# Weights of the second network: split during attention, or split in the routing head and the first expert

## The reference, cut to what matters

```python
for t in range(S):                              # _attn_ref: B, H, S, D = 4, 8, 768, 48
    cur = np.einsum('bhd,bhe->bhde', u[None] * kt, vt)
    y[:, :, t] = np.einsum('bhd,bhde->bhe', rt, state + cur)
    state = w[None, :, :, None] * state + np.einsum('bhd,bhe->bhde', kt, vt)
x = y.transpose(0, 2, 1, 3).reshape(3072, 384)
# _moe_ref: 8 experts take 384 tokens each, in the order of falling logits
for e in range(8):
    out[mask] = np.maximum(x[mask] @ w1[e], 0.0) @ w2[e]      # 384x1024, 1024x384
# _moe2_ref, on every token
h = np.maximum(x @ w_in, 0.0)                   # 384x2048
return h * h @ w_out                            # 2048x384
```

## Time and profile before

| | |
|---|---|
| median of 3 executions | 878.4 us (878.37 to 878.81) |
| the profiled execution | 878.33 us |
| its span, from first to last instruction | 876.6 us |
| mean granted clock of TensorE | 0.969 |
| attention, until the first routing instruction | 168.65 us |
| first matmul of the first expert | at 212.99 us |

### The profile page before, as it was taken

How to read it: one execution, slowest core, us unless ns; L and a number is a source line. 1 busy time by engine, 2 the same in 40 slices (tenths; PEclk the granted TensorE clock), 3 DMA queues, 4 the chain that set the end, 5 groups by cost and what they waited for, 6 DMA issues and landing times.

```text
span 876.6 us, 18438 instructions
## 1 busy us (share of the span) xinstructions
PE 811.8 (93%) x6695; PEld 777.4 (89%) x6695; DVE 551.1 (63%) x1159; ACT 290.0 (33%) x581; POOL 328.7 (37%) x312
## 2 busy tenths in 40 slices
PE   5999999624999999999999999999999999999995
PEld 4888888623899999999999999999999999999995
DVE  7999999675777458546845692678358633931210
ACT  1233332103135315422542253235314533542332
POOL 6777677203026303520541063126303520531232
PEclk9999999855999999999999999999999999999998
DMA  8776776013023001200310040022002200400000
GB/s 228 213 220 232 214 250 209 29 51 121 2 73 100 26 2 72 99 27 0 120 50 27 8 162 0 27 72 99 9 18 72 99 27 1 172 1 28 1 1 27
DMA packets 22143, 69.86 MB, mean 80 GB/s; under 512 B 3552, under 2 KB 6752, under 8 KB 22112
## 3 DMA queue, kind: packets, MB, share of 16 engines
q1 hardware_dynamic: 19040, 59.99, 21.2%
q0 software_dynamic: 3072, 9.44, 3.1%
HBM read 59.98 MB, written 9.44 MB: 79 GB/s over the span
## 4 chain that ended last, share of the span: by engine, by line
PE 77%; DVE 11%; issue 5%; POOL 5%; ACT 1%; DMA 0%; DVEq 0%; POOLq 0%
PE bank L1196 16%; PE bank L1197 15%; PE bank L1198 15%; PE bank L1250 8%; PE bank L1252 8%; PE bank L1251 8%; PE bank L1143 3%; DVE ks L638 2%; PE bank L1059 2%; DVE am L645 1%; DVE rs L639 1%; POOL rku L401 1%; DVE hot L802 1%; POOL kn L385 1%; POOL rk L396 1%
## 5 line engine op out<-in xcount | busy, mean ns | idle before, releaser
L469 POOL TENSOR_TENSOR h_lo<-sq,h_hi 128x384 fp32r<-128x384 f32 x128 | 152.9, 1198 | 398.2 <-DVE sq L966 398.1
L966 DVE SCALAR_TENSOR_TENSOR sq<-bank,relu 128x384 f32<-128x384 f32 x128 | 71.0, 555 | 133.6 <-ACT relu L565 133.3
L1250 PE MATMUL bank<-m_hi,h_hi 128*128 128x384 f32 x384 | 132.0, 344 | 0.0
L1196 PE MATMUL bank<-x_hi,m_hi 128*128 128x384 f32 x384 | 130.6, 340 | 0.3
L1252 PE MATMUL bank<-m_hi,h_lo 128*128 128x384 f32 x384 | 129.8, 338 | 0.0
L1251 PE MATMUL bank<-m_lo,h_hi 128*128 128x384 f32 x384 | 129.5, 337 | 0.0
L1197 PE MATMUL bank<-x_lo,m_hi 128*128 128x384 f32 x384 | 129.2, 336 | 0.0
L1198 PE MATMUL bank<-x_hi,m_lo 128*128 128x384 f32 x384 | 129.1, 336 | 0.0
L565 ACT ACTIVATE relu<-bank 128x384 f32<-128x384 f32 x128 | 63.0, 492 | 194.5 <-PE bank L1198 192.3
L559 ACT ACTIVATE h_hi<-bank 128x384 fp32r<-128x384 f32 x64 | 31.5, 492 | 192.1 <-PE bank L1198 192.0
L958 DVE SCALAR_TENSOR_TENSOR h_lo<-bank,h_hi 128x384 fp32r<-128x384 f32 x64 | 35.4, 554 | 72.0 <-ACT h_hi L559 72.0
(11 more groups left out here) (172 smaller groups left out, 1572.4 us busy)
## 6 DMA issues: line engine op xcount, KB each, us to landing
w_raw<-we_in SPq DMA_DIRECT2D x48, 512.0 KB, 4.9
nn<-nn_in SPq DMA_DIRECT2D x24, 576.0 KB, 4.1
tt<-tt_in SPq DMA_DIRECT2D x48, 192.0 KB, 4.9
m_raw<-m_in SPq DMA_DIRECT2D x12, 512.0 KB, 5.7
x_rows<-yrow SPq DMA_DIRECT2D x24, 192.0 KB, 1.9
xg<-x_rows,perm_next POOLq DMA_INDIRECT x24, 4.4
out<-xg,perm_now POOLq DMA_INDIRECT x24, 2.6
u_row<-u_in SPq DMA_DIRECT2D x1, 192.0 KB, 6.0
```

Of the source, the lines that this page charges most:

```text
L469: pool.tensor_tensor(h_lo[g % 3][:, :], sq[g % 2][:, :], h_hi[g % 3][:, :].bitcast(f32), ALU.subtract).then_inc(lo2_ready, 1)
L966: dve.scalar_tensor_tensor(out=sq[g % 2][:, :], in0=h_ps[g % 3][:, 0:CAP], scalar=0.0, in1=relu[:, :], op0=ALU.max, op1=ALU.mult).then_inc ...
L1196: pe.matmul(out, hi_w, hi_x, start=first, stop=False)
L1250: pe.matmul(acc_ps[t][:, 0:DM], h_hi[r][:, s], m2_hi[:, c:c + DM], start=first, stop=False)
```

## The change

The second network's tiles are no longer split in attention. All twelve are loaded once into a tile `m2_raw` that occupies the same memory as `m2_lo`, so that the low part is written over the loaded values. The six tiles of `w_in` are loaded after the last rows of attention are stored, the six of `w_out` after the loads of the first expert. The high parts are made by ScalarE: three before it splits the first expert's weights, three after its `x_high`, six at hidden tiles 2, 3, 4, 9, 10 and 11 of the first expert. The low parts of `w_in` are made by GpSimd: four as soon as `x_lo` is complete, two at hidden tiles 8 and 10. Those of `w_out` are made by VectorE at hidden tiles 8, 10, 13, 16, 18 and 21. TensorE waits for them where it first uses them. The first expert is written out ahead of the loops of GpSimd, ScalarE and VectorE.

```diff
+IN_TILES = [d * (F2 // WT) + f for f in range(F2 // WT) for d in range(DC)]
+OUT_TILES = list(range(DC * F2 // WT, M2_TILES))
+IN_LOW_AT = {8: 4, 10: 5}
+OUT_HIGH_AT = {2: 0, 3: 1, 4: 2, 9: 3, 10: 4, 11: 5}
+OUT_LOW_AT = {8: 0, 10: 1, 13: 2, 16: 3, 18: 4, 21: 5}
...
+        m2_raw = sb("m2_raw", [P, M2_TILES * WT], f32, loaded)
+        loaded.close()
+
         m2_lo = sb("m2_lo", [P, M2_TILES * WT], f32r)
...
+        def m2_high(eng, j):
+            cols = slice(j * WT, (j + 1) * WT)
+            eng.wait_ge(m2_loaded[j], 16)
+            return eng.activation(m2_hi[:, cols], m2_raw[:, cols], ACT.Copy)
+        def m2_low(eng, j):
+            cols = slice(j * WT, (j + 1) * WT)
+            return eng.tensor_tensor(m2_lo[:, cols], m2_raw[:, cols], m2_hi[:, cols].bitcast(f32), ALU.subtract)
...
-                elif b < 3:
-                    load_m2(b - 1, b - 1)
...
-                    if not last and b % 2:
-                        sp.wait_ge(m2_lo_ready, 4 * i + b + 1)
-                        load_m2(b // 2, 2 * i + b // 2 + 2)
...
+            for j in IN_TILES:
+                load_m2(j)
             sp.wait_ge(logit_ready, NU)
             load_expert(0)
+            for j in OUT_TILES:
+                load_m2(j)
...
+            def in_low(n):
+                pool.wait_ge(in_hi_ready, n + 1)
+                m2_low(pool, IN_TILES[n]).then_inc(in_lo_ready, 1)
+            pool.wait_ge(x_lo_ready, DC)
+            for n in range(len(IN_TILES) - len(IN_LOW_AT)):
+                in_low(n)
...
                     if not last and g == GATHER_AT:
                         gather(i + 1)
+                    if is_first(i) and g in IN_LOW_AT:
+                        in_low(IN_LOW_AT[g])
...
-                    if b % 2 and not (last and b == B - 1):
-                        m2_high(2 * i + b // 2 + 1, 1 - b // 2, i + 1 + b // 2)
...
+            for j in IN_TILES[0:DC]:
+                m2_high(act, j).then_inc(in_hi_ready, 1)
             for j in range(W1_TILES + 1):
                 split_high(0, j)
             for d in range(DC):
                 x_high(0, d)
+            for j in IN_TILES[DC:]:
+                m2_high(act, j).then_inc(in_hi_ready, 1)
...
                     high(i, g)
+                    if is_first(i) and g in OUT_HIGH_AT:
+                        m2_high(act, OUT_TILES[OUT_HIGH_AT[g]]).then_inc(out_hi_ready, 1)
...
-                    m2_low(i, b)
...
+            def out_low(n):
+                dve.wait_ge(out_hi_ready, n + 1)
+                m2_low(dve, OUT_TILES[n]).then_inc(out_lo_ready, 1)
...
+                        if is_first(i) and g in OUT_LOW_AT:
+                            out_low(OUT_LOW_AT[g])
...
                 pe.wait_ge(masked, 2 * n + 2)
+                pe.wait_ge(nn_in[b], 16 * i + 16)
...
+                        if (g - G1) * P % WT == 0 and d == 0:
+                            pe.wait_ge(in_lo_ready, DC * ((g - G1) * P // WT + 1))
...
                     pe.wait_ge(lo2_ready, G2 * i + g - G1 + 1)
+                    tiles = [-(-k * DM // WT) for k in (g - G1, g - G1 + 1)]
+                    if tiles[0] < tiles[1]:
+                        pe.wait_ge(out_lo_ready, tiles[1])
...
-            pe.wait_ge(m2_lo_ready, 2 * M2_TILES)
```

More of the change, by code:

```diff
@@ L106, in build @@
         m2_hi = sb("m2_hi", [P, M2_TILES * WT], f32r)
+        loaded = ExitStack()
+        m2_raw = sb("m2_raw", [P, M2_TILES * WT], f32, loaded)
+        loaded.close()
         m2_lo = sb("m2_lo", [P, M2_TILES * WT], f32r)
@@ L153, in build @@
         wg = sb("wg", [P, DC, E], f32, att)
-        m2_raw = [sb(f"m2_raw{j}", [P, WT], f32, att) for j in range(2)]
         att.close()
@@ L225, in build @@
         inter_done = sem("inter_done")
-        m2_in = [sem(f"m2_in{j}") for j in range(2)]
         scores_ready, masked, update_ready, z_ready = sem("scores_ready"), sem("masked"), sem("update_ready"), sem("z_ready")
@@ L231, in build @@
         yT_sum, yT_ready, logit_sum, logit_ready = sem("yT_sum"), sem("yT_ready"), sem("logit_sum"), sem("logit_ready")
-        m2_hi_ready, m2_lo_ready = sem("m2_hi_ready"), sem("m2_lo_ready")
+        m2_loaded = [sem(f"m2_loaded{j}") for j in range(M2_TILES)]
+        in_hi_ready, in_lo_ready = sem("in_hi_ready"), sem("in_lo_ready")
+        out_hi_ready, out_lo_ready = sem("out_hi_ready"), sem("out_lo_ready")
         y_stored = [sem(f"y_stored{b}") for b in range(B)]
@@ L278, in load_nn, with load_m2 @@
                 sp.dma_start(nn[b][:, :, :], nn_d[bass.ds(n, 1), :, :, :].rearrange("o p a f -> p (o a) f")).then_inc(nn_in[b], 16)
-            def load_m2(j, n):
-                sp.dma_start(m2_raw[j][:, :], m2_d[bass.ds(n, 1), :, :].rearrange("o p f -> p (o f)")).then_inc(m2_in[j], 16)
+            def load_m2(j):
+                sp.dma_start(m2_raw[:, j * WT:(j + 1) * WT], m2_d[j, :, :]).then_inc(m2_loaded[j], 16)
             sp.wait_ge(w_gap, 1)
@@ L481, in expert @@
                     keep_perm(i + 1)
-            with pool.Fori(0, E - 1) as i:
+            expert(0, False)
+            with pool.Fori(1, E - 1) as i:
                 expert(i, False)
@@ L492, in _ @@
             act.sem_inc(out_ready, TT)
-            def m2_high(m, j, times):
-                act.wait_ge(m2_in[j], 16 * times)
-                act.activation(m2_hi[:, bass.ds(m * WT, WT)], m2_raw[j][:, :], ACT.Copy).then_inc(m2_hi_ready, 1)
             def turned_y(n):
@@ L526, in units @@
                         gated(n - 1)
-                    if b % 2 and not (last and b == B - 1):
-                        m2_high(2 * i + b // 2 + 1, 1 - b // 2, i + 1 + b // 2)
-            m2_high(0, 0, 1)
             units(0, False)
@@ L589, in _ @@
                 split_high(0, j)
-            with act.Fori(0, E - 1) as i:
+            expert(0, False)
+            with act.Fori(1, E - 1) as i:
                 expert(i, False)
@@ L665, in state_sum @@
                                   u_ps[0:HD, 0:PAIRS * D].rearrange("p (q f) -> p q f", q=PAIRS), ALU.add).then_inc(z_ready, 1)
[L667 to L673, removed]
             def rows(i, b):
@@ L1024, in _ @@
                 split_low(dve, 0, j)
-            with dve.Fori(0, E - 2) as i:
+            expert(0, False, True)
+            with dve.Fori(1, E - 2) as i:
                 expert(i, False, True)
```

## The result

The changed kernel takes 880.5 us (median of 8 executions, 880.27 to 881.53), the kernel before 878.4 (8 executions, 878.29 to 878.81): ratio 1.0027, 95% interval 1.0016 to 1.0037. It is 2.1 us slower; 882.4 was predicted, in a range of 877.5 to 886.0. The executions fall into two groups, five at 880.3 to 880.5 and three at 881.5. The profiled one is of the upper group (881.5 us, span 879.8, mean clock 0.961), so its trace accounts for 3.2 us more than the span before, not for 2.1. The mean clock of the lower five is 0.964, of the upper three 0.961, 0.961 and 0.963.

What follows compares the result with a forecast made beforehand. Attention was taken as bound by a VectorE-GpSimd chain containing `m_lo`, with TensorE the busy engine from the routing head on. Terms: 5.2 + 2.3 + 4.8 + 0.6 - 8.9 = +4.0 us on 878.4, so 882.4 us, range 877.5 to 886.

Steps and rivals of the forecast that it cites:

- likeliest case: The forecast itself, chance 0.58: attention gains, the first expert loses more, 882.4 us; alone it reaches from 880.3 to 885.
- attention: Attention units: without `m_lo` TensorE becomes the bound, gaining 8.9 us (8.1 to 9.4).
- routing head: Routing head: input loads and three `m_hi` fall in ScalarE's idle time; cost 0.
- wait for `h_lo` at the start: First expert's start: GpSimd's four subtractions hold VectorE, so TensorE idles 6.2 us instead of 1.0; +5.2 us (4.7 to 5.9).
- first fall of the clock: First expert's start: TensorE's long idle drops its clock to 0.50, with a slow return; +2.3 us (0 to 3.4).
- second half, VectorE's chain: First expert's second half: two GpSimd and two VectorE pieces delay the next expert's list; +4.8 us (2.5 to 6).
- `h_lo` of tile 15: First expert's second half: GpSimd's `h_lo` behind the late gather comes late; +0.6 us (0 to 1.5).
- the rival with the full clock: First expert's start: the chip does not count the 6.2 us as idle, clock stays full; 880.1 us, chance 0.17.
- the bound over VectorE and GpSimd: Attention unit: the chain over both engines without `m_lo` would take 6.35 - 0.56 = 5.79 us.
- the rule that VectorE is held for the sum of GpSimd's pieces: First expert's start: VectorE's two-input work waits out GpSimd's four pieces, 2.28 us each, 9.1 us, until 223.0.
- GpSimd lets VectorE through: First expert: GpSimd's subtractions are held up instead of holding VectorE, start costs 0, no clock fall; 870 us, chance 0.12.
- attention does not shorten: Attention: units stay at 6.35 us because `rku` goes before `ks`; 891 us, chance 0.08.

Runs made afterwards that it cites:

- e5: Changed kernel with 42 extra matmuls (results unused) keeping TensorE busy ahead of its second `contract` of the first expert; 880.0 us.
- e1: Changed kernel with GpSimd's four input-tile subtractions at the first expert's start moved to VectorE's wait for the gathered rows; 876.3 us.
- e6: Changed kernel with only VectorE's first two output pieces moved, from hidden tiles 8 and 10 to 4 and 5; 878.7 us.
- e4: Kernel before with VectorE's attention subtraction `m_lo` replaced by a one-input reduction over as many values, low parts left out; 869.2 us.
- e7: Changed kernel with only GpSimd's last two input pieces (hidden tiles 8 and 10) moved to VectorE's wait for the gathered rows; 876.8 us.
- e10: Changed kernel rearranged: VectorE's `w_lo` wait for the first gather's landing; GpSimd splits two input tiles afterwards, VectorE four by tile 7, outputs from tile 4; 867.6 us.
- e3: Changed kernel with four input pieces on VectorE before the gathered rows, two on GpSimd after keeping the row list, first two output pieces at tiles 4, 5; 870.4 us.
- e9: Kernel before with one line more: VectorE's three `w_lo` ahead of the first expert wait until the first gather has landed; 876.9 us.
- e11: e10 with the first `w_lo` moved from GpSimd, where it ran beside `hot`, to VectorE behind `hot`; 866.2 us.

## Why the prediction was right, and where its sizes were off

The likeliest case happened, at its lower edge. By its steps, for the profiled execution:

| step | predicted | measured | from |
|---|---|---|---|
| attention | -8.9 | -9.0 | shift at the first tile |
| routing head | 0 | 0 | same |
| wait for `h_lo` at the start | +5.2 | +4.7 | e5: -9.0 to -4.3 |
| first fall of the clock | +2.3 | +1.3 | e5 against the changed kernel, fourth tile |
| second half, VectorE's chain | +4.8 | +4.6 | starts of TensorE, -3.0 to +1.6; the same in e1 and e5 |
| `h_lo` of tile 15 | +0.6 | 0 | no wait there; 0.5 in e1, e5 and e6, where the clock stays full |
| second fall of the clock | none | +1.6 | starts of TensorE, +1.6 to +3.2 |
| sum | +4.0 | +3.2 | spans 879.8 and 876.6 |

That the trace comes as near as 0.8 us to the forecast is luck in part: the second fall, which the forecast did not have, makes up for terms that were too large. Without it the measured steps are -9.0, +4.7, +1.3 and +5.1, in all +2.1, which is also the difference of the medians. The stated range held; the sum was 1.9 us too high. The median of 880.5 lies only 0.4 us from the 880.1 of the rival with the full clock; it is the trace that decides against that rival, not the time.

**Attention** went as worked out: `ownv` 0.83 us, 5.86 us per unit, TensorE the bound. e4 shows the reason: an instruction of the same length with one input costs nothing. Of the bound over VectorE and GpSimd (5.79 us) nothing can be said, since TensorE's lies above it.

**The start**: the rule that VectorE is held for the sum of GpSimd's pieces held. 5.2 was too much by 0.5 because I counted all of VectorE's time behind 208.7 us as blocked; `best` with one input runs beside the last piece (0.34 us), so that much was not lost. The rest I leave unexplained.

**The clock**: the likeliest case was right that it falls, and 2.3 us for it was the mis-sized term. It is at 0.50 from 217 to 223.8 us, but TensorE stands idle until 218.5 of that. Both traces begin the second `contract` there, and until the end of the group for tile 3 the changed kernel's matmuls are slower by 2.0 us: the nine of the `contract` take 3.05 us in place of 1.71, the group of tile 3 takes 2.68 in place of 2.00. But in e5 TensorE waits for VectorE's `hot` between the two (0.36 us in the line shown; with the matmuls that follow it 0.7 us), and the changed kernel comes too late to wait. 2.0 less 0.7 is the 1.3. The second fall was not in the forecast at all: three waits of 1.71, 0.76 and 1.24 us within 14 us, ahead of a fall at 268.2. It comes and goes: e1 and e5 have the same waits for VectorE, and their profiled executions do not have it; what decides it stays open. The Trainium skill's page TensorE: Matmul & The Clock Gate (section HAM oscillation), by which a wait between blocks of matmuls can make the next block start cold, agrees with the changed kernel's trace at the first place, where one wait of 5.17 us stands ahead of the slow matmuls. The three shorter waits of the second place are not the case which that section describes.

**The second half**: 4.6 us against 4.8, and its division was right in place: 1.9 us at the ranks, 2.4 at the ids, and 0.4 ahead of both, which the sum did not have: VectorE's piece at tile 8 holds GpSimd's `h_lo`. The sum took 4.56 us of GpSimd's pieces and 2.28 of VectorE's together, less 1.4 of idle time and 0.65 of slack. By the same sum GpSimd's alone would cost 2.5 us (3.1 with the `h_lo` of tile 15) and VectorE's alone 0.2; measured are 3.4 and 0.7 (e6, e7), so each alone was set too low and the two together too high. The 0.6 for the `h_lo` of tile 15 is there as 0.5 in e1, e5 and e6; in the changed kernel's trace TensorE comes there late by its fallen clock and does not wait.

**The rivals.** That GpSimd lets VectorE through is refuted by `gt` at 2.33 us and `pre` at 2.40. That attention does not shorten is refuted by its 5.86 us; the order of `ks` and `rku` did not flip. That the clock stays full did not happen, but e5, in whose trace it does, has its fastest executions at 879.0 to 879.3, where that rival had been given 880.1.

## What to carry to other kernels

Where VectorE and GpSimd both work on SBUF, count the two as one resource. On VectorE's side this held here for instructions with two SBUF inputs and for `gt`, whose second input is a column of scalars, but not for reductions; on GpSimd's side for its subtractions, for a small copy and for the issue of a gather. Look for a short instruction that lasts as long as its neighbour on the other engine. Where VectorE has such work waiting, a piece on the idle GpSimd costs VectorE twice what the same piece costs on VectorE itself (2.3 us against 1.14 for 128x1024), so moving it pays only where VectorE has nothing of this kind to do, and the same goes for VectorE beside the issue of a gather. An edit that wins time in a balanced stage must put its work where the engine it holds is waiting: the same twelve subtractions cost 12 us in the first expert as placed by the change (2.9 of it by the clock), and nothing in e10, where the shift stays at -10.8.

## What the runs showed of the hardware that I had not expected

**VectorE holds the issue of GpSimd's indirect transfers.** Beside VectorE's two-input `w_lo` the issues take 2.05 and 1.77 us, beside `m_lo` 1.97 (e3); with VectorE idle they take 1.15, 0.95 and 0.95 (e9). One line that makes VectorE wait is worth 1.5 us in the kernel before.

**A small instruction is held as long as a large one.** `gt`, a TENSOR_SCALAR of 128x24 with a column of scalars, took 2.33 us beside GpSimd's `m_lo`, and a GpSimd copy of 128x3 took 1.02 to 1.11 us beside VectorE's `w_lo` (e9, e10, e11; 0.18 us otherwise). Reductions, with one input, were not held: `best` took 0.34 us beside `m_lo`, and `scrap` of e4 0.68 beside `ownv`.

**The two engines take turns.** At the start of the changed kernel the four GpSimd pieces took 2.38, 2.38, 3.38 and 3.32 us and VectorE's two `w_lo` 1.93 and 3.42: each of the last two pieces waited for one `w_lo` of 1.1 us, and the second `w_lo` waited for one piece of 2.3.

**The same waits do not always bring a fall of the clock.** The changed kernel's trace has one from 268.2 to 271.6 us, which costs 1.1 us net; the traces of e1 and e5 have the same waits for VectorE and no fall. That equal executions of one kernel differ in this way is likely by the two groups of the changed kernel, 1.2 us apart with mean clocks of 0.964 and 0.961 to 0.963, but not shown: each kernel has one trace.
